# Attention with top-32 selection and two feed-forward layers: the softmax of a step moved into the step of its selection

## The reference

```
scores = scale * q @ k^T                       # 4 batches, 8 heads, 576 x 576, head size 64
kth    = 32nd largest score of a row
scores = where(scores >= kth, scores, -1e9)
attn   = exp(scores - max) / (sum + 1e-9)
x      = attn @ v                              # rows of 8*64 = 512
```

## Time and profile before

| what | value |
|---|---|
| median of 3 runs | 1056.23 us |
| profiled execution | 1057.04 us |
| its span | 1054.8 us |
| TensorE (PE) busy | 992.9 us, 94% |
| VectorE (DVE) busy | 817.3 us, 77% |
| ScalarE (ACT) busy | 727.6 us, 69% |
| GpSimd (POOL) busy | 711.9 us, 67% |
| chain that ended last | TensorE 80%, VectorE 8%, GpSimd 4%, ScalarE 3%, issue 3% |

### The profile page before, as it was taken

The page is one execution under the profiler, slowest core; times in us unless marked ns, Lnnn a source line. Parts: engine busy times, 40 slices in busy tenths (PEclk is TensorE's granted clock), DMA queues, the critical chain, the costliest instruction groups (busy, mean ns, idle before and its releaser), DMA issues.

```text
span 1054.8 us, 21596 instructions
## 1 busy us (share of the span) xinstructions
PE 992.9 (94%) x6878; PEld 806.3 (76%) x6879; DVE 817.3 (77%) x1744; ACT 727.6 (69%) x1390; POOL 711.9 (67%) x831
## 2 busy tenths in 40 slices
PE   5565899999999999999999999999999999999996
PEld 2343687788788788788788888887887788888875
DVE  7999999999999999999999999994345622222261
ACT  3888898988998998998888999998554111111140
POOL 2688898889899899899888899899351311111101
PEclk9996899999999999999999999999999999999999
DMA  9723253343344343324434333333481421111100
GB/s 311 257 91 127 112 171 121 128 143 121 114 153 165 114 157 121 124 98 144 169 119 155 117 120 102 121 121 121 156 331 54 165 96 52 40 40 40 40 20 20
DMA packets 43391, 130.99 MB, mean 124 GB/s; under 512 B 4320, under 2 KB 18656, under 8 KB 33056
## 3 DMA queue, kind: packets, MB, share of 16 engines
q1 hardware_dynamic: 40256, 120.09, 32.5%
q0 software_dynamic: 3040, 9.70, 2.7%
HBM read 111.95 MB, written 18.09 MB: 123 GB/s over the span
## 4 chain that ended last, share of the span: by engine, by line
PE 80%; DVE 8%; POOL 4%; ACT 3%; issue 3%; DMA 1%; SPq 1%; ACTq 0%; DVEq 0%; POOLq 0%
PE psum L614 8%; PE psum L575 7%; PE psum L644 7%; PE psum L737 6%; PE psum L739 6%; PE psum L738 6%; PE psum L646 6%; PE psum L645 6%; PE psum L663 6%; PE psum L665 6%; PE psum L664 6%; PE psum L589 5%; DVE top L1158 3%; DVE work L1164 3%; PE psum L769 2%
## 5 line engine op out<-in xcount | busy, mean ns | idle before, releaser
L1158 DVE MAX8 top<-work 128x8 f32<-128x576 f32 x432 | 305.4, 752 | 0.0
L1164 DVE MATCH_REPLACE8 work<-top,work 128x576 f32<-128x576 f32 x288 | 212.6, 749 | 0.0
L644 PE MATMUL psum<-x_parts,wi_hi 128*128 128x256 f32 x576 | 171.1, 297 | 0.0
L645 PE MATMUL psum<-x_parts,wi_hi 128*128 128x256 f32 x576 | 162.9, 283 | 0.0
L646 PE MATMUL psum<-x_parts,wi_lo 128*128 128x256 f32 x576 | 162.7, 283 | 0.0
L614 PE MATMUL psum<-prT,vtok 128*64 128x128 f32 (+3 forms) x1600 | 117.1, 287 | 15.2 <-ACT prT L918 15.2
L614 PEld LDWEIGHTS psum<-prT,vtok 128*64 128x64 f32 (+1 forms) x1600 | 85.5, 144 | 54.2 <-issue 41.2
L575 PE MATMUL psum<-kT,qT 64*128 64x512 f32 (+3 forms) x640 | 113.0, 480 | 11.5 <-DMA qT<-in_q 4.4
L1638 POOL DMA_INDIRECT out<-ys,dst_now x19 | 19.2, 1012 | 152.6 <-DVE ys L1360 150.7
L663 PE MATMUL psum<-wo_ring,h_hi 128*128 x288 | 119.1, 414 | 1.0 <-POOL h_lo L1547 0.9
L1541 POOL TENSOR_TENSOR hs<-hs,ab 128x512 f32<-128x512 f32 x72 | 93.7, 1301 | 32.7 <-ACT ab L941 32.5
(11 more groups left out here) (215 smaller groups left out, 2353.1 us busy)
## 6 DMA issues: line engine op xcount, KB each, us to landing
wo_ring<-wo_parts SPq DMA_DIRECT2D x72, 1024.0 KB, 4.8
wo_parts<-wo_ring SPq DMA_DIRECT2D x8, 1024.0 KB, 3.8
kT<-in_k SPq DMA_DIRECT2D x16, 288.0 KB, 3.4
qT<-in_q SPq DMA_DIRECT2D x16, 288.0 KB, 3.9
vtok<-in_v SPq DMA_DIRECT2D x16, 256.0 KB, 2.9
wo_raw<-in_moe_w_out SPq DMA_DIRECT2D x1, 4096.0 KB, 14.1
wi_raw<-in_moe_w_in SPq DMA_DIRECT2D x4, 1024.0 KB, 14.4
x_rows<-x2tok SPq DMA_DIRECT2D x16, 256.0 KB, 2.4
```

What stands on the lines that cost most here:

```text
L644: nc.tensor.matmul(ps[:, part, :], wi_hi[:, u, kk, f], hi, start=first, stop=False)
L645: nc.tensor.matmul(ps[:, part, :], wi_hi[:, u, kk, f], lo, start=False, stop=False)
L1158: nc.vector.max(top[:, at, 8 * r:8 * r + 8], sc_of(n)[:, t, :] if r == 0 else work[:, t, :]).then_inc(topk_step, 1)
L1164: nc.vector.match_replace(work[:, t, :], top[:, at, 8 * r - 8:8 * r], sc_of(n)[:, t, :] if r == 1 else work[:, t, :], TAKEN).then_inc(topk ...
```

## The change

It does the following.

* In the first stage ScalarE normalises block i-1 in step i instead of block i-2, behind the exponentials of the same step; the copy to prT moves to the front of the step, x_out and scores_out behind the exponentials. TensorE does the transposes and the product with v before the scores of a step. GpSimd makes the denominators of all blocks, VectorE's reduction goes.
* VectorE's reciprocal of block n-1 stands before the last two MAX8 of block n, in all blocks.
* In the second stage ScalarE's exponentials of a block move from the end of a step to the front of the next one, and h_high behind scores_out; the cut goes behind the copy to prT. GpSimd's biases of a block stand at the front of the next step, softplus, x_split, denominators and h_low at its end.
* Scores are made one step later in the second stage (block i+2 in step i), and step 9 makes none.
* Limits and maxima are one product on GpSimd with a table of two factors. The load of w_out is split into halves with a semaphore each. Block 8 gets both tiles masked with ScalarE's ramp.

ScalarE, one plain step of the second stage: in the first piece the step begins with h_high of the unit before (L949) in the code before. hs and ab are the softplus buffers, pr the probabilities, sc_more a slot of the scores ring.

The reciprocal moved ahead of the last two MAX8, and the reduction is gone. The diff, cut to its core:

```
-    FREE = MLP_AT - 2
+    FREE = MLP_AT - 1
...
-        wi_loaded, wo_loaded, wg_loaded = sem("wi_loaded"), sem("wo_loaded"), sem("wg_loaded")
+        wi_loaded, wg_loaded = sem("wi_loaded"), sem("wg_loaded")
+        wo_loaded = [sem("wo_loaded_0"), sem("wo_loaded_1")]
...
         def scores_at(i):
-            return i + 1 if i <= 0 else i + AHEAD
+            return i + 1 if i <= 0 else i + 3 if i < MLP_AT - 1 else i + 2 if i >= MLP_AT else BLOCKS
+
+        def scores_made(i):
+            return min(i + 4, MLP_AT + 2) if i < MLP_AT else min(i + 3, BLOCKS)
...
-            sp.dma_start(wo_raw[:], w_out.rearrange("(k p) n -> p k n", p=P)).then_inc(wo_loaded, 16)
+            for half in range(2):
+                at = slice(half * KF // 2, (half + 1) * KF // 2)
+                sp.dma_start(wo_raw[:, at, :], w_out.rearrange("(k p) n -> p k n", p=P)[:, at, :]
+                             ).then_inc(wo_loaded[half], 16)
...
@@ TensorE
+                if i < MLP_AT:
+                    if late:
+                        turn_probs(i - 2, scores_made(i - 1))
+                        times_v(i - 2)
+                    if is_block(n):
+                        scores(n, max(i - 1, 0))
...
@@ ScalarE, steps below MLP_AT
                     if late:
-                        normalise(i - 2, 0)
-                        normalise(i - 2, 1)
-                    if is_block(i - 3):
-                        x_out(i - 3)
+                        probs_out(i - 2)
                     if now:
                         for t in cuts(i - 1):
                             cut_off(i - 1, t)
-                    scores_out(scores_at(i))
                     if wo_unit(i) is not None:
                         split_wo(wo_unit(i))
+
                     if now:
                         exponentials(i - 1, 0)
+                    if late and i == MLP_AT - 1:
+                        x_out(i - 2)
+                    if now:
                         exponentials(i - 1, 1)
-                    if late:
-                        probs_out(i - 2)
-                    if wi_unit(i) is not None:
-                        split_wi(wi_unit(i))
+                    if late and i < MLP_AT - 1:
+                        x_out(i - 2)
+                    if is_block(scores_at(i)):
+                        scores_out(scores_at(i))
...
+                    if now:
+                        normalise(i - 1, 0)
+                        normalise(i - 1, 1)
+                    if wi_unit(i) is not None:
+                        split_wi(wi_unit(i))
...
@@ VectorE
             def reciprocals(n):
-                if n < MLP_AT - 1:
-                    dve.wait_ge(exp_ready, 2 * n + 2)
-                    nc.vector.tensor_reduce(den[:, n % 2, :], eps[:, n % 2], AX.X, ALU.add
-                                            ).then_inc(den_step, 1)
                 dve.wait_ge(den_step, n + 1)
+                if n >= 2:
+                    dve.wait_ge(pr_ready, 2 * n - 2)
...
-                    if r == 1 and n > MLP_AT:
-                        reciprocals(n - 2)
+                    if r == ROUNDS - 1 and n:
+                        reciprocals(n - 1)
...
@@ GpSimd
-                if cuts(n):
-                    nc.gpsimd.tensor_scalar(bias[:, n % 2, 1, :], top[:, at, TOPK - 1], FAR, None,
-                                            ALU.mult).then_inc(limit_ready, 1)
-                nc.gpsimd.tensor_scalar(bias[:, n % 2, 0, :], top[:, at, 0], -1.0, None,
-                                        ALU.mult).then_inc(bias_ready, 1)
+                nc.gpsimd.tensor_tensor(bias[:, n % 2], top[:, at, 0:TOPK:TOPK - 1].rearrange("p t x -> p x t"),
+                                        factors[:], ALU.mult).then_inc(bias_ready, 1)
...
+                now = is_block(i - 1)
+                if now:
+                    biases(i - 1)
+                if i < MLP_AT and is_block(i - 3):
                     x_split_up(i - 3)
...
+                if i < MLP_AT:
+                    if i == MLP_AT - 1:
+                        x_split_up(i - 2)
+                    if wo_unit(i) is not None:
+                        low_wo(wo_unit(i))
+                    if now:
+                        denominators(i - 1)
+                else:
+                    if up_at(i):
+                        softplus(*up_at(i))
+                    if is_block(i - 2):
+                        x_split_up(i - 2)
+                    if now:
+                        denominators(i - 1)
+                    if up_at(i):
+                        h_low(*up_at(i))
                 if wi_unit(i - 1) is not None:
                     low_wi(wi_unit(i - 1))
```

More of the change, by code:

```diff
@@ L305, in build @@
         topk_step, mask_step, masked = sem("topk_step"), sem("mask_step"), sem("masked")
-        cut, limit_ready = sem("cut"), sem("limit_ready")
+        cut = sem("cut")
         w1_first, w2_first = sem("w1_first"), sem("w2_first")
@@ L894, in cut_off @@
             def cut_off(n, t):
-                act.wait_ge(limit_ready, sum(1 for x in range(n + 1) if cuts(x)))
+                act.wait_ge(bias_ready, n + 1)
                 if n >= 2:
@@ L1060, in _ @@
                         scores_out(scores_at(i) + 2)
-                    continue
+                    if now:
[3 more added lines that the diff above has]
+                        split_wi(wi_unit(i))
+                    continue
+                behind = late and i > MLP_AT
+                if behind:
+                    exponentials(i - 2, 0)
+                    exponentials(i - 2, 1)
+                if is_block(i - 3) and i > MLP_AT:
+                    x_out(i - 3)
+                if is_block(scores_at(i)):
+                    scores_out(scores_at(i))
                 if up_at(i - 1):
                     h_high(*up_at(i - 1))
-                if is_block(i - 3):
-                    x_out(i - 3)
-                if now:
-                    for t in cuts(i - 1):
-                        cut_off(i - 1, t)
-                if is_block(scores_at(i)):
-                    scores_out(scores_at(i))
-                if late:
+                if behind:
                     normalise(i - 2, 0)
@@ L1077, in _ @@
                     probs_out(i - 2)
+                if now:
+                    for t in cuts(i - 1):
+                        cut_off(i - 1, t)
                 if i in TURNS:
@@ L1588, in _ @@
             nc.gpsimd.memset(scan_mask[:, :, 0:1], 0.0).then_inc(consts, 1)
+            pool.wait_ge(factors_ready, 2)
             for i in range(TAIL):
-                if i >= MLP_AT and is_block(i - 3):
+                now = is_block(i - 1)
+                if now:
+                    biases(i - 1)
+                if i < MLP_AT and is_block(i - 3):
                     x_split_up(i - 3)
-                if up_at(i - 1):
-                    h_low(*up_at(i - 1))
-                if is_block(i - 1):
+                if now:
                     for t in tiles_of(i - 1):
                         mask(i - 1, t)
-                if i < MLP_AT and is_block(i - 3):
-                    x_split_up(i - 3)
+                if i < MLP_AT:
[3 more added lines that the diff above has]
+                        low_wo(wo_unit(i))
+                    if now:
+                        denominators(i - 1)
[4 more added lines that the diff above has]
+                        x_split_up(i - 2)
+                    if now:
+                        denominators(i - 1)
+                    if up_at(i):
+                        h_low(*up_at(i))
                 if wi_unit(i - 1) is not None:
                     low_wi(wi_unit(i - 1))
-                if wo_unit(i) is not None:
-                    low_wo(wo_unit(i))
-                if up_at(i):
-                    softplus(*up_at(i))
-                if is_block(i):
-                    biases(i)
-                if is_block(i - 1) and i - 1 >= MLP_AT - 1:
-                    denominators(i - 1)
-            x_split_up(BLOCKS - 1)
-            h_low(LASTG - 1, UNITS - 1)
             for u in range(5):
```

37 lines of the change are left out of this document (18 added, 19 removed).

## The result

The changed kernel takes 1062.40 us (median, 1060.64 to 1062.91), the kernel before 1056.23 us on the same chip: ratio 1.0055, 95% interval 1.0043 to 1.0067. It is slower by 6.2 us. The prediction was 1062, from a sum of +6.2; not all of its terms were right. The profiled execution took 1062.0 us, its span is 1060.3.

A forecast was written before the change was run, and what follows sets the result against it. VectorE's selection paces the first stage, TensorE the second with VectorE nearly full. Terms -2.1 + 0.3 + 3.6 + 1.4 + 1.2 + 1.8 = +6.2, rounded to 6, give 1063 from 1057.0, 1062 as a median; range 1056 to 1067.

The forecast's parts named there:

- The ring behind the denominators: First stage: normalise, transposes, prT copy, cut, masks, low_wo, denominators; 10.5 us a block, or 9.8 with fast transposes.
- R(3): Start of VectorE's reciprocal inside block 3, first stage; forecast at 47.0 us, set by wi_raw landing at 38.72.
- R(9): Start of VectorE's reciprocal inside block 9, end of the first stage; forecast at 107.7 us.
- R(8): Start of VectorE's reciprocal inside block 8, first stage; forecast at 98.0 us, bounds 96.0 and 99.8.
- slow bound: First stage: late limit of 99.8 us for R(8), five periods taking 52.7 us at the slow pace of the transposes.
- The third rival: First stage: TensorE's transposes stay at 1.2 GHz; +7.8 us in all, 1064; chance 0.13.
- The passage: Into the second stage: last low_wi on GpSimd delays block 10's masks; step 13 still starts 2.1 us earlier than before.
- P(13): Moment TensorE begins step 13, start of the second stage's steps; forecast at 136.5 us, before 138.6.
- (a): First steps of seven groups, second stage: h_high now stands ahead of normalise; +0.51 us each, 3.6 in all.
- (c): Step 69, second stage: the scores of block 71 move there from step 68, one more product; +1.2 us.
- (d): Steps 70 to 73, end of the second stage: VectorE's blocks of 9.70 us hold TensorE; +1.8 us.
- (b): Plain steps of the second stage: slack shrinks from 0.6 to 0.1 us, 0.23 lost a group; +1.4 in all.

The follow-up runs named there:

- e4: Changed kernel with h_high ahead of scores_out in groups' first steps, last low_wi between block 9's masks, denominators ahead of low_wo in the first stage; 1055.56 us.
- e6: Changed kernel with needless identity products keeping TensorE busy in the first stage; 1060.61 us, ratio 1.0037.
- e1: Changed kernel with h_high ahead of scores_out in the first step of each group; 1058.05 us, ratio 1.0013.
- experiments 5 and 6: Needless TensorE products in the first stage: in the changed kernel 1060.61 us, in the kernel before 1054.76; with further edits e10 1052.05, e9 1051.37.
- e9: Changed kernel with the three edits of e4, needless TensorE products in the first stage, and second-stage scores one step earlier; 1051.37 us, ratio 0.9954.
- e10: Changed kernel with the three edits of e4 and needless TensorE products in the first stage; 1052.05 us, ratio 0.9964.
- e7: Changed kernel with scores made one step earlier in the second stage, as in the kernel before; 1061.62 us, ratio 1.0039.
- e3: Changed kernel with the denominators ahead of low_wo on GpSimd in the first stage; 1059.84 us, ratio 1.0038.

## Why the prediction was right, step by step

- *First stage.* The ring behind the denominators is there, with the period worked out for the slow pace: 10.5, and the waits 0.65 to 0.84. But the prediction missed the second ring, found with e4, that has the same 10.49 us at the slow pace. In the changed kernel the two arrive together: ScalarE's scores_out waits 0.47 for TensorE, and normalise, right behind it at 58.16, starts as the reciprocal of 57.94 is done.

```profile
57.03 0.28 ACT L904 ACTIVATE sc<-psum 128x128 f32<-128x128 f32 x1 [0.47 <-PE psum L585]
...
57.94 0.17 DVE L1195 RECIPROCAL rden<-den 128x2 f32<-128x2 f32 x1 [0.68 <-POOL den L1535]
...
58.16 1.45 ACT L928 ACTIVATE pr<-pr,rden 128x576 f32<-128x576 f32 x2
```

  Each was seen alone: the predicted one where the scores were faster (e6 above; e1 with scores of about 2.0 us, 10.21 a block and waits of normalise of about 0.28 for the reciprocal), the second one in e4. R(3) = 47.46 against 47.0 was luck. It was put down to the landing of wi_raw, but ScalarE waits only 0.18 us for it (38.83), and the copy to prT at 40.31 waits for TensorE; the periods are 10.45 and 10.48 already from R(1) = 26.53. Wrong was also the choice that the transposes become fast from the fifth block on. Eight take 1.94 us in six of the eight blocks seen before R(9), and the granted clock stood at 0.51 from 60 to 90 us, 0.79 before. R(8) came at 99.01, between forecast and slow bound. The third rival was thus half of the truth. The Trainium skill, "TensorE: Matmul & The Clock Gate", Part 1, has the half clock as the state after idling and the full one after sustained work; experiments 5 and 6 agree with it, since needless work alone brought the eight down to 1.23 in five of eight blocks (e6, e9) and six of eight (e10).
- *The passage.* The step that failed. Predicted R(9) + 28.8, measured R(9) + 30.5. The low_wi stands where it was put (122.46 against 120), and block 11 waits as predicted, 3.01 instead of about 2. From R(9) to the masks of block 10 were forecast 14.6 us, and it took 16.4; from there to P(13) the walk was right (14.2, measured 14.1). In the trace the delay runs through TensorE, which was not counted: transposes of block 8 wait 1.59 for scores_out of block 12 (112.69), the scores of 13 at 117.59 take 1.72 and hold ScalarE 0.83. That is read from the trace and not shown by an experiment; e7 takes away the wait of 1.59, and the low_wi still starts 13.5 us after R(9), 13.7 in the changed kernel. With 1.0 from R(8), the gain of 2.1 became a loss of 0.7. So of the signs that the prediction named, step 13 near 136.5 did not come.
- *(a)* exact in sum and shown by e1. *(c)* exact as an interval, but not as a cause of its own: by e7 (c) and (d) are one thing, 2.5 us by which VectorE's blocks of 9.70 end late, of which only 0.45 goes with the place of the scores. Predicted 3.0; why VectorE ends late against the kernel before stays open for the other 2.0.
- *(b)* was wrong: the plain steps of five groups take 9.39 to 9.50, those of the group of step 50 take 9.76 (before 9.81), and none of 9.6 to 9.7 stands before a group's end. The walk had a slack of 0.1 us and a ring of 9.5 built from a dozen starts rounded to 0.1; that is no basis for a loss of 0.2 a group.
- The sum hit because errors cancelled. Up to P(74) the terms measured are 0.7 - 0.2 + 3.6 + 0 + 1.2 + 1.2 = +6.5: the passage came out 2.8 worse, (b) 1.4, (d) 0.6 and the steps 13 to 17 0.5 better than forecast. It cannot be claimed that the whole was understood to 0.3 us.

## What to carry to other kernels

When a step of a pipeline of engines is moved earlier, list what now stands between its input and its output on every engine, small casts too: 0.5 us in front of a critical instruction was paid seven times in full, and cost nothing where the engine waited anyway. An engine that looks half idle can set the pace by its clock; where its operations appear at two durations in the trace, work out each ring at both and see which the new order leaves. Undo parts one at a time and then together: the sum of the single gains (8.5 us) against the joint one (5.7) pointed to a second ring; the slow blocks of e3 alone had shown it already.

## What the runs showed of the hardware

- Eight transposes of 128x128 took 1.94, 1.23 or 1.06 us, the product with v 2.60 or 1.46, the scores 2.40 or 1.30. The granted clock from 60 to 90 us was 0.51 (1.2 GHz) in the changed kernel, where the three blocks there had the long durations, and 1.00 (2.4 GHz) in e9 with the short ones. From 60 to 90 us TensorE worked 20.42 us at the slow pace in e4, 22.31 with the needless products at the fast one in e9.
- The granted clock of a window is no sure sign of the pace. e4 has 1.00 from 60 to 90 us with transposes of 1.94:

```profile
60.00:90.00 30.00, 20.42 (x109) 13.68 (x107) 28.01 (x61) 25.08 (x44) 23.96 (x24) 1.00 0.25 103
```

  The durations tell it, since the changed kernel has 0.51 there with the same 1.94. Nor does the mean clock of an execution order the times: e4's slowest (1057.41 us) has 0.993, its fastest (1052.99) 0.972. Why the records differ stays open.
- The executions of e4 and e7 spread over 4.4 and 3.8 us, those of e9 and e10, kept mostly fast, over 1.8 and 1.4. It fits that the blocks with the fast pace change from one execution to the next, but each kernel left one trace only, so that is not shown.
